# Answers of a gated linear attention kept channels-first on TensorE, their last two heads put in place by small transfers, and a new order of the work on VectorE, ScalarE and GpSimd

## What is computed

```python
def _attn_ref(q, k, v, a_re, a_im):          # B, H, S, D = 4, 8, 768, 48
    mag = np.sqrt(a_re * a_re + a_im * a_im)
    scale = np.minimum(mag, 0.999) / (mag + 1e-06)
    a_re_n, a_im_n = (a_re * scale, a_im * scale)
    for t in range(S):
        new_re = ar * S_re - ai * S_im
        new_im = ar * S_im + ai * S_re
        S_re, S_im = (new_re + kv, new_im)   # kv: outer product of k[t] and v[t]
        y[:, :, t] = np.einsum('bhd,bhde->bhe', q[:, :, t], S_re)

def _moe_ref(x, w1, w2, w3, w_out):          # x 3072 x 384, w1..w3 384 x 768
    h = np.maximum(np.maximum(x @ w1, x @ w2), x @ w3)
    return h @ w_out

def _moe2_ref(x, expert_emb, tau, w1, w2):   # 8 experts, 384 x 1024 and 1024 x 384
    expert_idx = np.argmax(logits, axis=1)   # one expert per token
    out[mask] = gate_w[mask, None] * (np.maximum(x[mask] @ w1[e], 0) @ w2[e])
```

## Time and profile before

| | |
|---|---|
| median of 3 runs | 1046.34 us |
| profiled execution, its own time | 1045.43 us |
| its span in the trace | 1043.3 us |
| TensorE (PE) busy | 888.8 us, 85% |
| VectorE (DVE) busy | 639.8 us, 61% |
| ScalarE (ACT) busy | 447.8 us, 43% |
| GpSimd (POOL) busy | 471.4 us, 45% |
| mean granted clock of TensorE | 0.938 of full |

### The profile page before, as it was taken

How to read it: one execution, slowest core, us unless ns; L and a number is a source line. 1 busy time by engine, 2 the same in 40 slices (tenths; PEclk the granted TensorE clock), 3 DMA queues, 4 the chain that set the end, 5 groups by cost and what they waited for, 6 DMA issues and landing times.

```text
span 1043.3 us, 18182 instructions
## 1 busy us (share of the span) xinstructions
PE 888.8 (85%) x6398; PEld 815.3 (78%) x6399; DVE 639.8 (61%) x1042; ACT 447.8 (43%) x810; POOL 471.4 (45%) x872
## 2 busy tenths in 40 slices
PE   0425677879899989999999999984999999999995
PEld 0324666769888978899999999974888888888785
DVE  5798767876778668767756745427633252537722
ACT  4643454435555525555334443222423243445621
POOL 1057795699785926992994000003212222223321
PEclk9999887888999969899999999995999999999998
DMA  9103144414233313313111111303711123324410
GB/s 293 55 19 87 55 107 120 102 68 125 80 87 83 90 41 94 79 50 86 34 46 48 34 41 34 137 17 136 271 47 45 38 89 115 120 76 158 158 38 30
DMA packets 37636, 89.59 MB, mean 86 GB/s; under 512 B 4008, under 2 KB 19120, under 8 KB 36160
## 3 DMA queue, kind: packets, MB, share of 16 engines
q1 hardware_dynamic: 33472, 76.30, 24.1%
q0 software_dynamic: 4096, 12.40, 3.8%
HBM read 70.20 MB, written 18.48 MB: 85 GB/s over the span
## 4 chain that ended last, share of the span: by engine, by line
PE 63%; DVE 18%; issue 6%; POOL 6%; ACT 3%; DMA 2%; DVEq 0%; ACTq 0%; SPq 0%; POOLq 0%
PE mm L1471 8%; PE mm L1472 7%; PE mm L1475 7%; PE yu L1471 4%; PE tr L1471 4%; PE tr L1475 4%; PE tr L1472 4%; PE yu L1472 4%; PE yu L1475 4%; PE sc L1528 3%; PE mm L1699 3%; PE yu L1571 2%; PE yu L1550 2%; PE yu L1559 2%; POOL c_im L1781 2%
## 5 line engine op out<-in xcount | busy, mean ns | idle before, releaser
L1471 PE MATMUL mm<-up_hi,x_hi 128*128 128x384 f32 x432 | 157.7, 365 | 9.5 <-ACT x_hi L695 6.2
L1472 PE MATMUL mm<-up_lo,x_hi 128*128 128x384 f32 x432 | 149.6, 346 | 0.0
L1780 POOL TENSOR_TENSOR c_re<-ring 112x128 f32<-112x128 f32 (+1 forms) x161 | 99.2, 616 | 102.3 <-DVE ring L984 57.8
L1028 DVE TENSOR_TENSOR h_sb<-mm,h_sb 128x384 f32<-128x384 f32 x96 | 53.1, 554 | 111.6 <-PE mm L1475 109.3
L1863 POOL DMA_INDIRECT out_rows<-g_o,rows_out x30 | 34.7, 1156 | 184.1 <-DVE g_o L1407 184.1
L868 ACT ACTIVATE g_h<-tr 128x512 f32<-128x512 f32 x60 | 35.9, 598 | 170.8 <-PE tr L1475 170.2
L1781 POOL TENSOR_TENSOR c_im<-ring 112x128 f32<-112x128 f32 (+1 forms) x161 | 104.4, 648 | 0.0
L1475 PE MATMUL mm<-up_hi,x_lo 128*128 128x384 f32 x432 | 100.9, 342 | 0.0
L1471 PEld LDWEIGHTS mm<-up_hi,x_hi 128*128 128x128 f32 x432 | 83.7, 194 | 12.9 <-issue 6.5
L1472 PEld LDWEIGHTS mm<-up_lo,x_hi 128*128 128x128 f32 x432 | 84.2, 195 | 0.0
L1783 POOL TENSOR_TENSOR ring<-c_re,c_im 112x64 f32<-112x64 f32 (+1 forms) x161 | 78.3, 486 | 12.6
(11 more groups left out here) (219 smaller groups left out, 2093.6 us busy)
## 6 DMA issues: line engine op xcount, KB each, us to landing
...
a_dn<-in_a_laid SPq DMA_DIRECT2D x20, 384.0 KB, 7.3
an_scratch<-a_dn SPq DMA_DIRECT2D x20, 384.0 KB, 2.3
ring<-an_scratch SPq DMA_DIRECT2D x20, 384.0 KB, 5.9
...
v_in<-in_v_laid SPq DMA_DIRECT2D x24, 192.0 KB, 2.7
x_scratch<-x_sb SPq DMA_DIRECT2D x24, 192.0 KB, 1.9
```

The source lines that it names most:

```text
L1028: nc.vector.tensor_tensor(hh, mm[:, (3 * half + w) % 2, 0:FH], hh, ALU.max).then_inc(p_maxed, 1)
L1471: nc.tensor.matmul(out, hi[:, x, :], w_hi(x), start=(x == 0), stop=False)
L1472: nc.tensor.matmul(out, hi[:, x, :], w_lo(x), start=False, stop=False)
L1780: nc.gpsimd.tensor_tensor(c_re[:, 0:count, :, :], cur, bc(prev[:, :, 0, :], 2, 2), ALU.mult).then_inc(chain_prod, 1)
```

## The change

- `answers`: `v_in` is now the stationary operand and `att` the moving one, so the output has channels on partitions. Even heads go to output partitions 0 to 63 (64 columns of `v_in` are taken, 48 of this head and 16 of the next), odd heads to 64 to 111. The part of the state uses `st_t` as the stationary operand and `q_t` as the moving one and follows at once in the same function; `answers_state` is gone. y takes one PSUM bank, the state's contribution (`outer`) the other.
- `moe_xt` is gone from the pipeline. ScalarE copies heads 6 and 7 to `y_end` and heads 0 to 5 to `x_raw`, which leaves two gaps of 16 partitions in each of three tiles; SP then moves `y_end` into the gaps with 6 transfers of 16 partitions x 128 (`move_x`), ahead of what else it has in the next iteration. The host lays the rows of w1, w2, w3 out to match. `outer` no longer waits for `x_lo`, `answers` no longer for `add_state`.
- `SINGLE` is 6: groups 4 and 5 get chains of 15 steps and 3 joins each, as groups 2 and 3.
- The order on VectorE, ScalarE and GpSimd changes: other iterations for the joins, the second `norm_m2` and `norm_square` behind `mask` and `x_hi`, `norm_sum` and `norm_mag` later, `up_low` spread, `turns` at other steps of the chains, the router's products at the start over two banks.

Cut to its core (the fallback path of single steps, the declarations and the body of `router` are left out):

```diff
-SINGLE = 4
+SINGLE = 6
@@ SP
+            def move_x(n):
+                sp.wait_ge(y_copied, 2 * (n + 1))
+                for x in range(KX):
+                    for b in range(2):
+                        sp.dma_start(x_raw[HALF * b + D:HALF * (b + 1), x, :], y_end[HALF * b + x * GAP:HALF * b + (x + 1) * GAP, :]).then_inc(x_moved, 16)
...
             for n in range(NC):
                 if n >= 1:
+                    move_x(n - 1)
                     for m in norms_in(n - 1):
                         store_unit(m)
...
+            move_x(NC - 1)
             sp.wait_ge(z_staged, 3 * NC)
             load_expert(0, 0)
@@ ScalarE
             def y_copy(n):
                 act.wait_ge(y_done, n + 1)
-                wait(act, xt_done, n)
-                nc.scalar.activation(y_sb[:, :].rearrange("p (h b d) -> p b h d", h=HP, b=2),
-                                     yu[:, :, 0:YW].rearrange("p b (h d) -> p b h d", h=HP), ACT.Copy).then_inc(y_copied, 1)
+                wait(act, xt_ready, n)
+                nc.scalar.activation(y_end[:, :], yu[0:R, 0, KX * P:FREE], ACT.Copy).then_inc(y_copied, 1)
+                nc.scalar.activation(x_raw[0:R, :, :], yu[0:R, 0, 0:KX * P].rearrange("p (k t) -> p k t", t=P), ACT.Copy).then_inc(y_copied, 1)
             def moe_x_hi(t):
-                act.wait_ge(xt_done, t + 1)
+                act.wait_ge(x_moved, 32 * KX * (t + 1))
...
+                late_z = n in joins_early
                 if prev:
                     moe_x_hi(n - 1)
                 if prev2:
                     moe_h_hi(n - 2)
-                if more:
+                for m in norms[1:]:
+                    norm_square(m, norm_of(m))
+                if more and not late_z:
                     stage_z(n + 1)
                     z_square(n + 1)
                 if prev2:
                     moe_out(n - 2)
+                for m in norms:
+                    norm_mag(m, norm_of(m))
                 if now:
                     kp_copy(n)
+                if more and late_z:
+                    stage_z(n + 1)
+                    z_square(n + 1)
...
                 if now:
                     y_copy(n)
-                for m in later[1:]:
-                    norm_square(m, norm_of(m))
-                for m in later:
-                    norm_mag(m, norm_of(m))
@@ VectorE
-            joins_early = {1: 1, 3: 2, 7: 4}
-            joins_late = {4: 3, 8: 5, 10: 6, 11: 7, 14: 8, 15: 9, 18: 10, 19: 11}
+        joins_early = {1: 1}
+        joins_late = {2: 2, 4: 3, 6: 4, 8: 5, 10: 6, 11: 7, 14: 8, 15: 9, 18: 10, 19: 11}
+                apart = 0 if n in (2, 10) else 1
...
-                    join(late, 0)
+                    for number in range(apart):
+                        join(late, number)
...
-                for m in later:
+                for m in later[:1]:
                     norm_m2(m, norm_of(m))
                 if prev:
                     moe_max(n - 1, 1, 1)
@@ TensorE
             def answers(n):
                 pe.wait_ge(masked, 2 * (n + 1))
-                pe.wait_ge(x_ready, n + 1)
+                wait(pe, y_copied, 2 * n)
+                alone = n % CB == 0
                 for h in range(HP):
                     for b in range(2):
-                        last = nc.tensor.matmul(yu[:, b, h * D:(h + 1) * D], att[:, b, h, :], v_in[:, (2 * h + b) * D:(2 * h + b + 1) * D],
-                                                start=(h == 0), stop=(n % CB == 0 and h == HP - 1))
+                        at = (2 * h + b) * D
+                        wide = slice(0, HALF) if b == 0 else slice(HALF, R)
+                        last = nc.tensor.matmul(yu[wide, 0, h * P:(h + 1) * P], v_in[:, at:at + (HALF if b == 0 else D)], att[:, b, h, :],
+                                                start=(h == 0), stop=(alone and h == HP - 1))
+                if not alone:
+                    pe.wait_ge(t_ready, n - n // CB)
+                    for h in range(HP):
+                        for x in range(2):
+                            for b in range(2):
+                                rows = rows_of(b)
+                                last = nc.tensor.matmul(yu[rows, 0, h * P:(h + 1) * P], st_t[rows, x, h, :], q_t[n % 2][rows, x, h, :],
+                                                        start=False, stop=(x == 1 and h == HP - 1))
...
-                if prev:
-                    moe_xt(n - 1)
...
                 if now:
                     answers(n)
                 if prev:
-                    moe_up(n - 1, range(3, 4))
-                if now:
-                    answers_state(n)
-                if prev:
-                    moe_up(n - 1, range(4, 6))
+                    moe_up(n - 1, range(3, 6))
@@ GpSimd
             for g in range(SINGLE, NG, 2):
                 if g > SINGLE:
                     turns(g - 2)
-                chain_steps(g, range(1, 13))
+                chain_steps(g, range(1, 17))
                 turns(g - 1)
-                chain_steps(g, range(13, HALF // 2))
+                chain_steps(g, range(17, HALF // 2))
```

149 lines of the change are left out of this document (85 added, 64 removed).

## The result

The changed kernel takes 1057.6 us (median of 7 runs, 1051.0 to 1059.6) against 1045.8 us (7 runs, 1043.9 to 1046.5): 1.0106 of the time before, 95% interval 1.0078 to 1.0134. The forecast was 1004.0 us, from 988 to 1030. It was wrong in sign. The seven times of the changed kernel lie apart: two at 1051, five from 1056.6 to 1059.6, so a difference against it is uncertain by some us.

The account below looks back on a forecast made before the run. Late iterations were taken as bound by TensorE's work, early ones by chains through VectorE and GpSimd. Gains 13.8 + 5 + 9 + 4 + 12 + 5 less 6.5 make 42.3 us; 1045.4 - 42.3 + 0.9 = 1004.0 us, range 988 to 1030.

Parts of the forecast that it names:

- TensorE's work per iteration: Transposes of y, answers and state on TensorE: 3.06 us against 4.25, 1.19 us less per iteration.
- The rival without side-by-side tiles: Column tiles of answers and state do not overlap: 1.3 us more per iteration, 1033 us; chance 0.07.
- the one with weight loads between the passes: Weight loads stand between the scores' passes: 0.53 us more per iteration, 1010 us; chance 0.15.
- 12 x 1.15 = 13.8 us: TensorE's saving, counted only where it sets the pace: iterations 8, 11, 12 and 15 to 23.
- y's new way, at nothing: The six small transfers of y on SP are hidden, with 0.3 us of cover before TensorE needs `h_hi`.
- the fourth rival: Small transfers land late and hold ScalarE's `h_hi`, then TensorE: slower, 1085 us at 7.3 us per landing; chance 0.06.
- Start, 5 us: Before iteration 1: shorter router work on ScalarE and one `up_low` moved into VectorE's idle time gain 5 us.
- Iterations 1 to 5, 9 us: VectorE's second `norm_m2` leaves the path to `moe_max`, for which TensorE waits: net gain 9 us.
- 6 and 7, 4 us: Iteration 7 loses two early joins ahead of `mask`, iteration 6 gets three: net gain 4 us.
- Iteration 10, 12 us: VectorE's joins no longer hold `moe_max` and `add_state` while waiting for GpSimd: 35.0 to 22.8 us.
- Against, 6.5 us: Put back for two more joins, a `norm_mag` ahead of `kp_copy`, and GpSimd's chains: 6.5 us.
- The reordering only moves the waits: VectorE's work and GpSimd's chains bind again one iteration later: 1023 us; chance 0.15.

Follow-up runs that it names:

- The filler: Changed kernel with `x_hi` behind `h_hi` (ScalarE), `x_lo` behind the mask (VectorE), half the scores computed twice in iterations 8 to 16; 1037.84 us.
- reorder_only: Kernel before with the new order alone; answers, states and transposes of y as before, no small transfers; 1040.65 us.
- joins_ahead: Changed kernel with `x_hi` behind `h_hi` (ScalarE), `x_lo` behind the mask (VectorE), two late joins ahead of `norm_sum`; 1025.54 us.

## Why the prediction was wrong, step by step

- **TensorE's work per iteration: right.** 0.92 + 1.84 + 0.3 was reckoned and 1.01 + 1.89 measured, with no extra for changing tiles beyond the first product's 0.45 us. The rival without side-by-side tiles and the one with weight loads between the passes both fell: that one wanted 1.45 us for the scores' part, and the rows have 1.01. The rule behind it (the Trainium skill, TensorE: Matmul & The Clock Gate, "The mechanism") is not borne out here.
- **"12 x 1.15 = 13.8 us": wrong.** The gain is real only in n=16 to 23. Where TensorE waits for VectorE I wrote that it "would wait longer for the same thing", at no price. The longer wait has a price, the granted clock, and the stretches behind iterations 7, 9 and 14 lost some 3 us each by it. The filler gave that back. With the wait at `x_hi` mended, the answers are worth 0 us in two orders and 1.9 in the best.
- **"y's new way, at nothing": the term that was mis-sized.** The end of the copies at E - 1.9 and TensorE's need for `h_hi` at E + 3.1 were right (601.93, and 607.85 less the wait of 0.86, with E = 603.84). The issue was not: 0.35 us, from issues over 112 to 128 partitions, against 0.61 for one of 16 partitions, 1.6 us more for six. The landing was right, 1.8 us against 1.9, though the queue has a smaller transfer than the 192 KB that I named as its smallest (128 KB at the start, 7.3 us). `x_hi` starts at E + 3.0 and `h_hi` ends at E + 3.9, 1.1 us later than reckoned, against 0.3 of cover. With the 16 iterations of the fourth rival that is 13 us; measured are 17 in the new order and, by the medians, 21 in the old one. Why an issue of this shape takes longer no run shows.
- **Start, 5 us: too low.** 9.7 us at n=1.
- **Iterations 1 to 5, 9 us; 6 and 7, 4 us: wrong in sign.** From n=1 to 7 `reorder_only` lost 6.0 us. I took early joins as standing in the way of the mask and late ones as nearly free. It is the other way round: early ones fill the wait for TensorE, late ones come on top of VectorE's bound stretch.
- **Iteration 10, 12 us: half right.** 33.6 to 28.0 in `reorder_only`; with the joins ahead, 21.4. Iterations 9 and 13 gained nothing.
- **Against, 6.5 us: GpSimd's part was not due in this order.** In `reorder_only` VectorE waits 0.22 us for GpSimd in iteration 14 and the stretch behind takes 23.3 us (22.9 before); n=7 to 14 is only 2 us shorter there than before. In `joins_ahead` it is 6 us shorter, and the wait is 7.06 and the stretch 30.0.
- **Rivals.** "The reordering only moves the waits" (0.15) was true of the order. "The transfers come late" (0.06) was true of the answers, by the issue and not by the landing: TensorE waited for `h_hi` in 11 of 24 iterations, where its sign wanted most, and I wanted 2.9 us of lateness for it: that was reckoned against 42 us of gain which was not there. I priced each rival with all other terms intact; two of them held together.
